# Reordering the start stage of a fused attention and two-layer MLP kernel

## The reference, cut to what matters

```
# attention: batch 4, heads 8, seq 768, head_dim 64; chunks of 32 queries, each sees
# 8 memory keys + 16 keys to the left + its own 32 + 8 to the right (a window of 64 keys)
scores = scale * q_c @ k_full.T;  scores -= max;  a = exp(scores);  a /= sum(a) + 1e-9
out_c  = a @ v_full
x = out as (3072 tokens, 512)
# first layer: 512 -> 1024 -> 512
h  = x @ w_in;  e = exp(h - max(h));  solu = h * e / (sum(e) + 1e-9)
ln = (solu - mean) / sqrt(var + 1e-6) * g_ln
x  = ln @ w_out
# second layer: 512 -> 2048 -> 512
out = leaky_relu(x @ w_in2, 0.01) @ w_out2
```

## Time and profile before

| | us |
|---|---|
| median of 3 runs (825.97 to 826.15) | 826.12 |
| the profiled execution, its own time | 827.22 |
| its span in the trace | 825.4 |
| PE busy in the span | 807.1 (98%) |
| DVE, ACT, POOL busy | 544.7, 455.5, 98.4 |
| granted TensorE clock, mean | 0.998 of full speed |

### The profile page before, as it was taken

One profiled execution on the slowest core, in us unless ns is written; L12 is line 12 of the kernel. 1 busy time (PEld: TensorE's weight loads), 2 busy tenths in 40 slices (PEclk: granted clock), 3 DMA queues, 4 the chain that ended last, 5 costly groups with the idle time before them and its releaser, 6 DMA issues.

```text
span 825.4 us, 13059 instructions
## 1 busy us (share of the span) xinstructions
PE 807.1 (98%) x4844; PEld 659.3 (80%) x4844; DVE 544.7 (66%) x898; ACT 455.5 (55%) x729; POOL 98.4 (12%) x220
## 2 busy tenths in 40 slices
PE   8889999999999999999999999999899999999998
PEld 7667878777888888888888888888678888888886
DVE  7778988877743286427643335455788699769775
ACT  4567777767743346345565446565644554555553
POOL 4444445442210000000000000000000000000000
PEclk9999999999999999999999999999999999999999
DMA  9675768664758876256684567545941840373002
GB/s 334 249 260 161 212 194 241 179 202 122 212 197 229 310 263 242 102 178 208 230 286 169 181 225 256 179 165 167 338 172 47 292 173 26 92 267 125 27 1 76
DMA packets 84496, 156.64 MB, mean 190 GB/s; under 512 B 6737, under 2 KB 35537, under 8 KB 84433
## 3 DMA queue, kind: packets, MB, share of 16 engines
q1 hardware_dynamic: 84432, 155.81, 56.5%
HBM read 99.16 MB, written 56.62 MB: 189 GB/s over the span
## 4 chain that ended last, share of the span: by engine, by line
PE 88%; DMA 3%; DVE 2%; issue 1%; POOL 1%; SPq 0%; ACT 0%; DVEq 0%; POOLq 0%
PE hid_a L732 21%; PE hid_b L732 20%; PE scores_a L732 13%; PE attn_ps L732 13%; PE scores_b L732 8%; PE probs_ps L732 7%; PE attn_ps L724 2%; PE probs_ps L710 1%; DMA g_blk<-g_scratch 1%; PE scores_b L698 1%; PE scores_a L698 1%; DMA g_scratch<-g_out 1%; DVE ring_lo L1127 1%; DVE g_blk L1263 1%; DMA q_raw<-q_in 0%
## 5 line engine op out<-in xcount | busy, mean ns | idle before, releaser
L858 ACT ACTIVATE ring_hi<-g_blk 128x512 fp32r<-128x512 f32 x168 | 105.9, 632 | 111.2 <-PE hid_b L732 40.6
L1127 DVE TENSOR_TENSOR ring_lo<-g_blk,ring_hi 128x512 fp32r<-128x512 f32 x168 | 115.4, 690 | 36.2 <-ACT ring_hi L858 33.0
L995 ACT ACTIVATE g_out<-g_out 128x512 f32<-128x512 f32 x72 | 45.4, 630 | 91.4 <-DVE g_out L1242 60.1
L732 PE MATMUL hid_b<-ring_hi,w_hi 128*128 128x512 f32 x128 | 50.2, 392 | 3.0 <-DVE ring_lo L1127 3.0
L732 PE MATMUL hid_b<-ring_hi,w_lo 128*128 128x512 f32 x128 | 49.9, 389 | 0.0
L732 PE MATMUL hid_b<-ring_lo,w_hi 128*128 128x512 f32 x128 | 49.8, 389 | 0.0
L732 PE MATMUL hid_a<-w_in_hi,xT_hi 128*128 128x512 f32 x96 | 39.9, 416 | 4.2 <-DVE u L1173 3.5
L732 PE MATMUL hid_b<-w_in_hi,xT_hi 128*128 128x512 f32 x96 | 39.3, 409 | 0.0
L732 PE MATMUL attn_ps<-x_op_P_hi,w_hi 128*128 128x512 f32 x96 | 37.7, 393 | 0.7 <-ACT g_out L858 0.7
L1127 DVE TENSOR_TENSOR x_op_P_lo<-op_raw,x_op_P_hi 128x1024 fp32r<-128x1024 f32 x21 | 25.7, 1224 | 18.9 <-ACT x_op_P_hi L858 18.8
L897 ACT ACTIVATE u<-u,shift,gain 128x1024 f32<-128x1024 f32 x24 | 29.7, 1238 | 15.0 <-POOL shift L1422 15.0
(11 more groups left out here) (205 smaller groups left out, 2150.2 us busy)
## 6 DMA issues: line engine op xcount, KB each, us to landing
g_scratch<-g_out SPq DMA_DIRECT2D x96, 256.0 KB, 2.4
g_blk<-g_scratch SPq DMA_DIRECT2D x48, 512.0 KB, 7.2
attn_buf<-k_in SPq DMA_DIRECT2D x32, 384.0 KB, 5.4
attn_buf<-v_in SPq DMA_DIRECT2D x32, 384.0 KB, 3.5
ln_scratch<-lnT SPq DMA_DIRECT2D x24, 512.0 KB, 5.7
w_raw<-w_in SPq DMA_DIRECT2D x16, 512.0 KB, 3.9
q_raw<-q_in SPq DMA_DIRECT2D x32, 192.0 KB, 5.1
ln_even<-ln_scratch SPq DMA_DIRECT2D x12, 512.0 KB, 7.0
```

Of the source, the lines that this page charges most:

```text
L732: mm = pe.matmul(psum, weights[i], data[j], start=first and n == 0, stop=last and n == 2, skip_group_check=goes_on)
L858: return act.activation(dst, src, ACT.Copy)
L995: act.activation(x, x, ACT.Prelu, alpha=0.01).then_inc(s_g[q], 1)
L1127: return ve.tensor_tensor(dst, x, hi.bitcast(f32), ALU.subtract)
```

## The change

It moves steps in `START` and nothing else: no step is added or dropped, and no wait, buffer or operand is changed. Engine by engine the order changes as follows (SP's order of loads stays the same).

The diff, without the lines that only pair the same steps otherwise:

```diff
         ("scores", 2), ("load_q", 6), ("load_k", 6), ("place_q", 3),
-        ("values", 0), ("load_v", 4), ("shift", 2),
-        ("probs_t", 1), ("x_hi", 0), ("spread", 1), ("x_lo", 0),
-        ("hidden", 0, 0), ("expo", 2), ("w1_hi", 1), ("rsum", 2),
-        ("values", 1), ("load_v", 5), ("w1_lo", 1), ("probs", 2),
-        ("scores", 3), ("load_q", 7), ("load_k", 7), ("x_hi", 1),
-        ("probs_t", 2), ("x_lo", 1),
-        ("hidden", 1, 0), ("spread", 2), ("shift", 3),
-        ("values", 2), ("load_v", 6), ("w1_hi", 2),
-        ("hidden", 0, 1), ("expo", 3), ("w1_lo", 2), ("x_hi", 2),
-        ("hidden", 1, 1), ("rsum", 3), ("w1_hi", 3), ("x_lo", 2), ("probs", 3),
+        ("probs_t", 1), ("shift", 2),
+        ("values", 0), ("load_v", 4), ("spread", 1), ("x_hi", 0), ("expo", 2), ("x_lo", 0), ("rsum", 2),
+        ("hidden", 0, 0), ("w1_hi", 1), ("probs", 2), ("w1_lo", 1),
+        ("values", 1), ("load_v", 5),
+        ("probs_t", 2), ("x_hi", 1),
+        ("scores", 3), ("load_q", 7), ("load_k", 7), ("spread", 2), ("x_lo", 1),
+        ("hidden", 1, 0), ("shift", 3), ("w1_hi", 2),
+        ("hidden", 1, 1), ("expo", 3), ("w1_lo", 2),
+        ("values", 2), ("load_v", 6), ("rsum", 3),
+        ("hidden", 0, 1), ("x_hi", 2), ("w1_hi", 3), ("x_lo", 2), ("probs", 3),
...
-        ("values", 4), ("load_v", 8), ("load_w1", 5), ("rsum", 5), ("expo1", 0),
-        ("scores", 7), ("load_q", 11), ("load_k", 11), ("neg_max", 1), ("probs", 5), ("x_hi", 4), ("place_q", 8),
-        ("probs_t", 5), ("rsum", 6), ("expo1", 1), ("stats_a", 0), ("solu", 0), ("spread", 5), ("probs", 6), ("shift", 7), ("stats_a", 1), ("square", 0),
-        ("hidden", 2, 0), ("place_q", 9), ("x_lo", 4), ("expo", 7),
-        ("probs_t", 6), ("solu", 1), ("stats", 0),
+        ("values", 4), ("load_v", 8), ("load_w1", 5), ("rsum", 5), ("expo1", 0), ("rsum", 6), ("probs", 5), ("x_hi", 4), ("solu", 0), ("place_q", 8),
+        ("probs_t", 5),
+        ("scores", 7), ("load_q", 11), ("load_k", 11), ("spread", 5), ("stats_a", 0), ("x_lo", 4),
+        ("hidden", 2, 0), ("square", 0), ("probs", 6), ("shift", 7), ("place_q", 9),
+        ("probs_t", 6), ("neg_max", 1), ("expo", 7),
...
```

More of the change, by code:

```diff
@@ L111 @@
         ("scores", 2), ("load_q", 6), ("load_k", 6), ("place_q", 3),
-        ("values", 0), ("load_v", 4), ("shift", 2),
-        ("probs_t", 1), ("x_hi", 0), ("spread", 1), ("x_lo", 0),
-        ("hidden", 0, 0), ("expo", 2), ("w1_hi", 1), ("rsum", 2),
-        ("values", 1), ("load_v", 5), ("w1_lo", 1), ("probs", 2),
-        ("scores", 3), ("load_q", 7), ("load_k", 7), ("x_hi", 1),
-        ("probs_t", 2), ("x_lo", 1),
-        ("hidden", 1, 0), ("spread", 2), ("shift", 3),
-        ("values", 2), ("load_v", 6), ("w1_hi", 2),
-        ("hidden", 0, 1), ("expo", 3), ("w1_lo", 2), ("x_hi", 2),
-        ("hidden", 1, 1), ("rsum", 3), ("w1_hi", 3), ("x_lo", 2), ("probs", 3),
-        ("hidden", 0, 2), ("w1_lo", 3), ("place_q", 4),
+        ("probs_t", 1), ("shift", 2),
[8 more added lines that the diff above has]
+        ("hidden", 0, 1), ("x_hi", 2), ("w1_hi", 3), ("x_lo", 2), ("probs", 3),
+        ("hidden", 0, 2), ("place_q", 4), ("w1_lo", 3),
         ("probs_t", 3), ("place_q", 5),
@@ L131 @@
         ("hidden", 1, 3), ("spread", 4), ("neg_max", 0), ("expo", 6),
-        ("values", 4), ("load_v", 8), ("load_w1", 5), ("rsum", 5), ("expo1", 0),
-        ("scores", 7), ("load_q", 11), ("load_k", 11), ("neg_max", 1), ("probs", 5), ("x_hi", 4), ("place_q", 8),
-        ("probs_t", 5), ("rsum", 6), ("expo1", 1), ("stats_a", 0), ("solu", 0), ("spread", 5), ("probs", 6), ("shift", 7), ("stats_a", 1), ("square", 0),
-        ("hidden", 2, 0), ("place_q", 9), ("x_lo", 4), ("expo", 7),
-        ("probs_t", 6), ("solu", 1), ("stats", 0),
-        ("values", 5), ("load_v", 9), ("load_w1", 6), ("spread", 6),
-        ("hidden", 2, 1), ("place_q", 10), ("rsum", 7), ("x_hi", 5), ("norm", 0), ("x_lo", 5), ("probs", 7),
-        ("hidden", 2, 2), ("square", 1), ("tr", 0), ("place_q", 11),
+        ("values", 4), ("load_v", 8), ("load_w1", 5), ("rsum", 5), ("expo1", 0), ("rsum", 6), ("probs", 5), ("x_hi", 4), ("solu", 0), ("place_q", 8),
[3 more added lines that the diff above has]
+        ("probs_t", 6), ("neg_max", 1), ("expo", 7),
+        ("values", 5), ("load_v", 9), ("load_w1", 6), ("spread", 6), ("stats", 0),
+        ("hidden", 2, 1), ("rsum", 7), ("x_hi", 5), ("place_q", 10), ("expo1", 1), ("x_lo", 5),
+        ("hidden", 2, 2), ("probs", 7), ("norm", 0), ("solu", 1), ("stats_a", 1),
         ("scores", 8), ("load_q", 12), ("load_k", 12),
-        ("values", 6), ("load_v", 10), ("shift", 8), ("place_q", 12), ("expo", 8), ("rsum", 8), ("w1_hi", 4), ("probs", 8),
+        ("values", 6), ("load_v", 10), ("place_q", 11), ("tr", 0), ("shift", 8), ("expo", 8), ("place_q", 12), ("square", 1), ("w1_hi", 4), ("rsum", 8), ("probs", 8),
 )
```

## The result

The changed kernel is slower: 826.71 us (median of 22 runs, 823.79 to 828.73) against 824.94 us (22 runs, 822.24 to 826.65). The ratio is 1.0025, with a 95% interval of 1.0016 to 1.0035. The three runs shown ahead of the prediction had a median of 826.12, 1.2 us above that of the 22. So 826.71 lies inside the predicted range of 824.5 to 827.6, but only because both were read against a kernel that seemed slower than it is. Against the median of the 22, the same range would have ended at 826.4. What was forecast, no change (825.9 against 826.12), didn't happen: the time moved clear of the noise, and the other way.

What follows compares the result with a forecast made beforehand. PE is busy from 63.6 to 420 us, so the start stage decides, through the landing of q 12. That landing's -0.2 gave 826.12 - 0.2 = 825.9 us, range 824.5 to 827.6.

Steps and rivals of the forecast that it cites:

- the walk of PE from hidden 0,0 to scores 6: PE, start stage: 15.04 us of work and a 0.4 us wait bring scores 6 at 32.5, 0.2 late.
- The rival that said just this: Start stage, from hidden 0,0: the clock falls behind PE's two idle times, 826.12 + 1.7 = 827.8 us; chance 0.12.
- One of the signs of being wrong: Clock column of the new trace: another stretch under 1.00 would show the prediction wrong.
- Its price: Loss from one low-clock stretch: 8 matmuls in 3.4 us that take 1.84 at full clock, so 1.6 us.
- that rival, which had 0.10: At 60.2 us: the lower clock doesn't come, 1.6 us saved, 824.3 us with the 0.2; chance 0.10.
- Load q 6: SP's load behind place_q 4, whose copies take 1.05 us: out at 26.7 instead of 27.01, -0.3, bound +1.2.
- The second part: Units 4 to 8: hidden 2,0 at 39.65 instead of 40.15 without waiting for solu 0; q 12 then decides.
- From q 12 to hidden 4,0: place_q 12 to hidden 4,0: 60.13 - 53.18 = 6.95 us of dependent work that the change doesn't touch.
- The landing: q 12 lands 8.2 us after its issue and sets hidden 4,0; the landing moves by 0.0 to -0.3, taken -0.2.
- Carried to the end: PE is busy from 63.6 to 420 us, so the start stage's gain or loss at 64 us reaches the end.
- The base: Median of the three runs, 826.12 us, 1.1 below the profiled execution's 827.22; the -0.2 was applied to it.

Runs made afterwards that it cites:

- the fitted kernel: The changed kernel with 6 warming matmuls behind scores 2 and 5 behind values 0: 825.00 us, 0.9998 to the kernel before.
- the swap alone: The kernel before with only probs_t 1 ahead of values 0 and spread 1 ahead of x_hi 0: 827.91 us, 1.0020.
- place_q 12 last: The kernel before with place_q 12 behind probs 8 and stats 1 in POOL's queue: 822.77 us, 0.9964.
- the first part alone: Kernel before plus the moves of probs_t 1, spread 1, probs_t 2 and hidden 1,1 ahead of values 0, x_hi 0, scores 3, values 2: 825.92 us, 1.0003.

## Why the prediction was wrong

**The step that failed** is the walk of PE from hidden 0,0 to scores 6: "17.03 + 15.04 + 0.4 = 32.5", made at full clock. hidden 0,0 came where it was forecast (17.12 for 17.0), with the idle times that were forecast (1.60 and 1.43 us for "3.0 us of 4.4"). But the clock fell there, in both traces of the changed kernel and, if the mean clock of 0.997 or less in 29 of its 34 listed executions is read that way, in most executions. scores 6 started at 34.42, and the delay went through scores 3, expo 3, probs 3 and place_q 4 to load q 6 (28.93 for 26.7). The rival that said just this was written down, with a chance of 0.12. What spoke for it in the rows was as strong as what spoke for the forecast: the only fall of the kernel before stood behind the same kind of stretch. I should have given it the larger chance. One of the signs of being wrong that the prediction named, another stretch of the clock column under 1.00, is what came. The walk itself was sound at full clock: in the fitted kernel scores 6 starts 0.3 us earlier than in the kernel before, counted from scores 2, where 0.2 later was forecast.

**Its price was too small as well.** I took 1.6 us, one stretch of 3.4 us at half clock. It was 6.8 us here, 5.78 of it busy. If half of a busy time at half clock is lost, that is 2.9 us, an estimate. Read from the traces it is 2.4: from scores 2 to scores 6 it takes 22.65 us, against 20.28 in the fitted kernel. The executions say 3.0: 827.2 us at 0.997 or less against 824.2 at 0.999 or more, though the latter are only four. Some of it is won back where the fall behind hidden 4,0 doesn't come: that rival, which had 0.10, came in both traces of the changed kernel and in the second one of the kernel before.

**Load q 6.** At full clock the step was right in sign and near in size (-0.46 for -0.3, in the fitted kernel). What decides it is that place_q 4 gets ahead of w1_lo 3: in the changed kernel too it starts at 27.86 and load q 6 goes out at 28.93, 1.07 us later, w1_lo 3 beginning at 28.82. The same gap of 1.07 us stands in the fitted kernel (copies from 25.21, load at 26.28), and where w1_lo 3 begins ahead of the copies, in the kernel before and in the swap alone, it is 1.9 us. The copies of place_q 5 then pay (3.10 us for the four, 3.03 in the fitted kernel).

**The second part** was right: hidden 2,0 loses its wait (in the changed kernel's trace PE waits 1.13 us ahead of probs_t 5, where 0.9 was forecast, and not ahead of hidden 2,0), and nothing arrives at the end (0.9999), since hidden 4,0 waits for q 12.

**From q 12 to hidden 4,0** the prediction had 6.95 us of untouched work from place_q 12; it is 62.02 - 55.08 = 6.94 after the change. It is 6.93 to 6.98 in all twelve traces in which place_q 12 has its old place, and taking the wait out of the way gave 1.9 us. The landing is another matter. It came 8.1 us after the issue, for 8.2, and that is luck: in the twelve traces it took 5.3 to 8.2 us, in the second trace of the kernel before 5.5. The prediction took this time as fixed. So hidden 4,0 differs by up to 2.7 us between executions of one kernel by the landing alone, and in single traces only the links up to load q 12 can be compared. What makes a landing slow stays open.

**From hidden 4,0 to the end.** "Carried to the end" held roughly. The span less the start of hidden 4,0, and less 1.6 us where the half clock stands behind it, is 763.4 to 765.3 us in all sixteen traces, so up to 1.9 us of a gain or loss at hidden 4,0 can still be evened out later. Between 420 and 800 us PE idles 4.4 us in the first trace of the kernel before and 5.6 in its second.

**The base.** The median of three runs was read as exact to 0.2 us. 22 runs put it 1.2 us lower, and executions of one kernel spread over 4 to 5 us, part of it with the clock and, by the traces, part with the landing of q 12. With place_q 12 last the nine executions spread over 2.4 us, those of the kernel before beside them over 4.9.

## What to carry to other kernels

Count idle time of TensorE not only by what it adds to the chain but by what it does to the clock behind it: swapping two steps for no gain at the place itself turned waits of 0.63 and 0.66 us into 1.60 and 1.43, and the half clock behind them cost some 2.4 us up to scores 6. Where an idle time can't be avoided, matmuls that nothing waits for kept the clock up in the start stage in all four traces that have them; their measured duration must fit the gap. And look in each queue for a step that waits for a transfer while ready work stands behind it: moving one copy behind two ready steps gained 0.36%, where the whole reordering lost 0.25%.

## What the runs showed of the hardware

- The granted clock in a given place differs between executions of one kernel. After a wait of 1.95 us at 60.13 us it fell to the lower level (1.2 GHz) for 3.4 us in one trace of the kernel before, and after 1.70 us at 58.37 us in another it stayed at the upper one (2.4 GHz). It also fell behind a wait of 1.57 us at hidden 2,0 in two traces (at 44.0 and 40.7 us), and stayed up behind one of 1.56 us there in a third. A trace with the clock up is no proof that it stays up.
- The low clock of the changed kernel lasted 6.8 us, although PE was busy for 5.78 of these. In the swap alone it lasted through 5.07 us of unbroken work (17.43 to 22.50 us), and with the first part alone it was over after some 3.4 us.
- A warming matmul of 128 x 128 in full fp32 counts as two in the trace and occupies PE for some 0.24 us at full clock: in the fitted kernel 10 entries, five matmuls, took 1.38 us, the drain of the last one included.
- One 192 KB load (q 12), issued at 44 to 50 us, took between 5.3 and 8.2 us to land in twelve traces, 5.5 and 8.2 in two executions of the same kernel. The DMA engines were 0.91 to 1.01 busy from 44 to 53 us in all of them, so their share doesn't tell the two apart.
